# A fused attention and two feed-forward layers on one core: the first batch written out per engine

## What is computed

```
attention, in chunks of 32 queries: context = 8 memory rows + 16 left + 32 own + 8 right
    scores = scale * q_c @ k_full.T ; a = exp(scores - max) / (sum + 1e-9) ; out = a @ v_full
x = out reshaped to 3072 x 512
SOLU layer:  h = x @ w_in (512 x 1024) ; solu = h * softmax(h) ; layer norm * g_ln ; @ w_out (1024 x 512)
second layer: h = x @ w_in2 (512 x 2048) ; g = h * clip(h + 3, 0, 6) / 6 ; @ w_out2 (2048 x 512)
```

## Time and profile before

| | |
|---|---|
| median of 3 runs | 938.34 us (937.13 to 939.4) |
| profiled execution | 938.23 us, span 936.4 us |
| TensorE busy, matmuls | 905.9 us (97%) |
| VectorE, ScalarE, GpSimd busy | 685.4, 473.2, 273.0 us |
| mean granted TensorE clock | 0.985 |
| chain that ended last | TensorE 80%, VectorE 13%, DMA 3%, ScalarE 2% |

### The profile page before, as it was taken

One profiled execution on the slowest core, in us unless ns is written; L12 is line 12 of the kernel. 1 busy time (PEld: TensorE's weight loads), 2 busy tenths in 40 slices (PEclk: granted clock), 3 DMA queues, 4 the chain that ended last, 5 costly groups with the idle time before them and its releaser, 6 DMA issues.

```text
span 936.4 us, 17274 instructions
## 1 busy us (share of the span) xinstructions
PE 905.9 (97%) x6200; PEld 812.0 (87%) x6200; DVE 685.4 (73%) x1094; ACT 473.2 (51%) x1092; POOL 273.0 (29%) x324
## 2 busy tenths in 40 slices
PE   7887999999999999999999999999999999999998
PEld 7666888988888888889988888888799999999997
DVE  3898687878777777866686555555788988878783
ACT  4645465555656564635675555455654333333320
POOL 5452165554432343552002332323550000000000
PEclk8987999999999999999999999999999999999999
DMA  9633326666644476458463333332987434344441
GB/s 191 149 67 63 93 53 178 180 179 171 190 141 137 100 219 165 139 175 334 170 254 128 116 138 123 142 127 111 351 315 270 137 101 149 114 141 135 130 137 45
DMA packets 146907, 146.46 MB, mean 156 GB/s; under 512 B 96936, under 2 KB 107176, under 8 KB 145832
## 3 DMA queue, kind: packets, MB, share of 16 engines
q1 hardware_dynamic: 134328, 100.55, 37.0%
q0 software_dynamic: 7920, 38.94, 11.5%
q10 hardware_dynamic: 4608, 6.29, 1.9%
HBM read 90.05 MB, written 55.71 MB: 156 GB/s over the span
## 4 chain that ended last, share of the span: by engine, by line
PE 80%; DVE 13%; DMA 3%; ACT 2%; issue 2%; SPq 0%; POOL 0%; DVEq 0%; POOLq 0%
PE banks L873 25%; PE banks L916 21%; PE banks L1057 21%; PE banks L827 3%; PE banks L840 2%; PE banks L864 2%; PE banks L796 2%; DVE prob L1317 2%; PE banks L853 2%; DVE gs_raw L1474 2%; DVE gs L1293 2%; DVE small L1313 1%; DMA k_in<-in_k_dram 1%; DMA ws<-w_split_scratch 1%; DVE score L1301 1%
## 5 line engine op out<-in xcount | busy, mean ns | idle before, releaser
L1057 PE MATMUL banks<-vs,gs 128*128 128x256 f32 x2016 | 243.3, 283 | 2.7 <-DVE o_stage L1507 1.5
L1057 PEld LDWEIGHTS banks<-vs,gs 128*128 128x128 f32 x2016 | 242.3, 192 | 3.8 <-DVE o_stage L1507 1.7
L916 PE MATMUL banks<-xs,ws 128*128 128x512 f32 x1008 | 230.5, 390 | 2.4 <-DMA ws<-w_split_scratch 1.8
L916 PEld LDWEIGHTS banks<-xs,ws 128*128 128x128 f32 x1008 | 188.3, 188 | 43.2 <-DMA ws<-w_split_scratch 2.2
L1253 ACT CAST gs<-gs_raw 128x1792 fp32r<-128x1792 f32 x48 | 81.6, 1700 | 132.2 <-DVE gs_raw L1474 132.1
L873 PE MATMUL banks<-y_t,w_out 128*128 128x384 f32 x768 | 140.8, 337 | 0.0
L873 PE MATMUL banks<-w_in,x_t 128*128 128x512 f32 x552 | 133.2, 397 | 1.1 <-DVE solu L1347 1.1
L873 PEld LDWEIGHTS banks<-y_t,w_out 128*128 128x128 f32 x768 | 132.2, 188 | 0.7
L873 PEld LDWEIGHTS banks<-w_in,x_t 128*128 128x128 f32 x552 | 103.1, 190 | 23.1 <-DVE solu L1347 1.4
L1105 ACT ACTIVATE prob<-score,small 96x128 f32<-96x128 f32 x256 | 99.8, 397 | 18.2 <-DVE small L1306 18.2
L1474 DVE TENSOR_TENSOR gs_raw<-gs_raw 128x256 f32<-128x256 f32 x192 | 82.6, 431 | 29.4 <-DMA gs_raw<-g_scratch 24.3
(11 more groups left out here) (88 smaller groups left out, 1077.4 us busy)
## 6 DMA issues: line engine op xcount, KB each, us to landing
g_scratch<-part SPq DMA_DIRECT2D x96, 256.0 KB, 2.0
gs_raw<-g_scratch SPq DMA_DIRECT2D x45, 512.0 KB, 3.9
q_in<-in_q_dram SPq DMA_DIRECT2D x32, 192.0 KB, 3.9
x_scratch<-x_out ACTq DMA_DIRECT2D x32, 192.0 KB, 2.0
out_dram<-o_stage SPq DMA_DIRECT2D x12, 512.0 KB, 5.7
k_in<-in_k_dram SPq DMA_DIRECT2D x24, 240.0 KB
v_in<-in_v_dram SPq DMA_DIRECT2D x24, 240.0 KB
v_split_scratch<-v_split POOLq DMA_DIRECT2D x3, 1792.0 KB, 7.7
```

The source lines that it names most:

```text
L916: mm = pe.matmul(ps, ws[:, W_OF[i], a, kc, :], xs[g][X_OF[i]][:, m, kc, :], start=(fresh and x == 0), stop=(x == len(passes) - 1), skip_gr ...
L1057: mm = pe.matmul(m_ps[i][:, s, :], gs[x][:, a, G_OF[i], s * P:(s + 1) * P], vs[p][:, m, V_OF[i], :], start=(p == 0 and s == 0 and y == 0), ...
```

## The change

Batch 0 no longer goes through `batch(b, first)`. Each engine gets a `first_batch()` with its pieces in an order of its own, by halves of a tile and by quarters of a product (`hidden_part`). Further:

- GpSimd scales the probabilities of attention tiles 0 to 6, one operation per head; later tiles are scaled by VectorE as before.
- All eight weight pieces have a buffer of their own (`w_first`, `w_later`, the latter where `y_t1` lies). GpSimd rounds all eight. VectorE subtracts for w_in 0 to 3. GpSimd subtracts for w_out in four quarters per piece.
- K's window 0 is loaded by ScalarE's queue. The weights and g_ln are asked for once that window is there. ScalarE makes one small copy early.
- `keep_busy` has 8 calls at the start and 8 near the end.
- Q loads wait for the turn of the Q before last, not for K's.

```diff
-        w_raw = at("w_raw", 184, [P, 2, PIECE], F32)
+        w_first = at("w_first", 184, [P, 2, PIECE], F32)
+        w_later = at("w_later", 112, [P, 6, PIECE], F32)
@@ GpSimd
+            def low_weights(p, x):
+                if x == 0:
+                    pool.wait_ge(w_hi_done, p + 1)
+                    pool.wait_ge(w_lo_done, p)
+                cs = slice(x * PIECE // 4, (x + 1) * PIECE // 4)
+                piece = nc.gpsimd.tensor_tensor(w_split_at(p, LO)[:, cs], w_piece(p)[:, cs],
+                                                w_split_at(p, HI)[:, cs].bitcast(F32), ALU.subtract)
+            def scale_half(n, half):
+                pool.wait_ge(srec_done, 2 * n + 1 + half)
+                for h in range(HB * half, HB * (half + 1)):
+                    last = nc.gpsimd.tensor_scalar(prob[:, h, :], prob[:, h, :], srec[:, h:h + 1], 1.0,
+                                                   ALU.mult, ALU.mult)
+                last.then_inc(prob_done, 1)
+            def first_batch():
+                pool.wait_ge(k_in_here[0], kv_here(0, 0))
+                    pool.dma_start(g_ln, moe_g_ln.rearrange("(c p) -> p c", p=P)).then_inc(g_ln_here, 16)
+                load_weights(0)
+                load_weights(1)
+                high_weights(0)
+                high_weights(1)
+                scale_half(0, 0)
+                load_weights(2)
+                scale_half(0, 1)
+                load_weights(3)
+                scale_half(1, 0)
+                scale_half(1, 1)
+                high_weights(2)
+                load_weights(4)
+                high_weights(3)
+                load_weights(5)
+                scale_half(2, 0)
+                scale_weights(4)
+                scale_half(2, 1)
...
+                low_weights(7, 3)
@@ TensorE
+                keep_busy(8)
+                turn_q(0, early_ps[0])
+                turn_k(0, early_ps[1])
+                turn_q(1, early_ps[0])
+                scores(0, True)
...
+                attend(0, 1, False)
+                scores(3, False)
+                hidden_part(0, 0)
+                hidden_part(0, 1)
+                turn_half(2, 0)
+                hidden_part(0, 2)
+                hidden_part(0, 3)
...
+                scores(6, False)
+                turn_half(5, 0)
+                keep_busy(8)
+                turn_half(5, 1)
+                turn_ln_half(1, 0)
+                attend(0, 5, False)
+                turn_ln_half(1, 1)
@@ ScalarE
+                load_window(act, k_in, k, mem_k, k_in_here, 0, 0)
+                act.wait_ge(three_ready, 1)
+                nc.scalar.copy(hsum, three)
+                copy_q(0, early_ps)
@@ VectorE
+            def first_batch():
+                mask_half(0, 0)
+                max_half(0, 0)
+                mask_half(0, 1)
+                low_weights(0)
+                den_half(0, 0)
+                max_half(0, 1)
+                rec_half(0, 0)
+                mask_half(1, 0)
+                max_half(1, 0)
+                den_half(0, 1)
+                rec_half(0, 1)
+                mask_half(1, 1)
+                max_half(1, 1)
+                low_weights(1)
...
+                low_x(0, 0, 0)
+                low_weights(2)
+                max_half(2, 1)
+                low_x(1, 1, 0)
+                low_weights(3)
...
+                low_x(5, 1, 1)
```

More of the change, by code:

```diff
@@ L552, in split_weights, with high_weights @@
+            def high_weights(p):
                 if p < WP1:
-                    hi, lo = (w_in[:, a, p, :] for a in (HI, LO))
+                    pool.wait_ge(w_raw_here[p % 2], 16 * (p // 2 + 1))
                 else:
[L555 to L560, removed]
@@ L726, in batch @@
                         mix_tokens(*{3: (0, 0), 5: (0, 1), 7: (1, 0)}[kk])
[L727 to L737, removed]
+            first_batch()
             batch(1, steps=0)
@@ L875, in split_products, with hidden_part @@
                 return mm
-            def hidden(i, u, par, first):
+            def hidden_part(m, x):
+                half, ks = x // 2, 2 * (x % 2)
+                if x == 0:
+                    if m > 0:
+                        pe.wait_ge(solu_done, m)
+                    pe.wait_ge(x_lo_done, m + 2)
+                if m == 0 and half == 0:
+                    pe.wait_ge(w_lo_done, ks + 2)
+                cols = slice(half * BANK, (half + 1) * BANK)
+                for kc in (ks, ks + 1):
+                    for y, (a, w) in enumerate(((HI, HI), (HI, LO), (LO, HI))):
+                        mm = pe.matmul(h_ps[:, cols], x_t[:, 0, a, kc, m * P:(m + 1) * P], w_in[:, w, kc, cols],
+                                       start=(kc == 0 and y == 0), stop=(kc == KD - 1 and y == 2))
+                if x == 3:
+                    mm.then_inc(h_done, 1)
@@ L1173, in batch @@
+            def batch(b, last=False):
                 for kk in range(TILES):
-                    w = work(kk, first, last)
+                    w = work(kk, last)
                     n = TILES * b + kk - 1
                     i, ii, u = 2 * b + kk // TPG, kk // TPG, kk % TPG
-                    if first and kk < TPG:
-                        copy_qk(kk, early_ps)
-                    if first and kk == 0:
-                        act.wait_ge(w_raw_here[0], 16)
-                        nc.scalar.copy(w_in[:, HI, 0, :], w_raw[:, 0, :]).then_inc(w_hi_done, 1)
@@ L1429, in _ @@
             dve.wait_ge(mask_ready, 1)
-            batch(0, first=True)
+            first_batch()
             with dve.Fori(1, B) as b:
```

635 lines of the change are left out of this document (471 added, 164 removed).

## The result

The changed kernel takes 950.86 us, the median of 4 runs (950.16 to 952.57). The kernel before took 938.85 us beside it (4 runs, 937.13 to 939.4). The ratio is 1.0134, 95% interval 1.0114 to 1.0154: 12 us slower, where 13 us faster was forecast.

A forecast was written before the change was run, and what follows sets the result against it. TensorE bounds after 100 us; before about 92 us VectorE is nearest to the bound. The walk's 19 us less 3 for port waits and 3 for clock give 13 won: 938.2 - 13 = 925 us, range 918 to 934.

The forecast's parts named there:

- after the gauge TensorE is full, so nothing gives the gain back: Rest of the kernel behind the first batch's start-up: all 13 us won earlier would last to the end.
- the gauge: Start of the fourth SOLU tile's product (tile 3) on TensorE, 91.27 us before; its earlier start measures the gain.
- the steady stretch unchanged in length: Sign to check in the dense TensorE part: its duration stays as before.
- The slower one, 944: GpSimd becomes the bound, halves queue behind weight work, all 13 us lost and 6 more; chance 0.09.
- The walk, 19.1 us: Following the five engines' written orders through the first batch up to tile 3's product: 19.1 us won.
- products 0 to 3: TensorE's products of SOLU tiles 0 to 3, walked to start at 28.7, 40.0, 51.1 and 72.2 us.
- Product 3 "near 77": Sign on TensorE: SOLU tile 3's product starts near 77 us with both deductions.
- rival 1: First batch: w_in 0 and 2 land late, or VectorE's subtractions wait for GpSimd; 7 us won, 931; chance 0.18.
- The port waits, 3 us: Deduction before batch 1: small VectorE operations wait for GpSimd at the SBUF port, 3 us, bounds 0 and 8.5.
- the point of failure: Sign on GpSimd: the prediction is wrong if a 96x128 scaling takes 0.5 us or more.
- The clock, 3 us: Deduction for TensorE at half clock over one product, one score set, one turned tile: 3 us, bounds 0 and 14.
- The w_out pieces: GpSimd's last w_out piece ends at 75.7 us, first projection wants it at 79.8: cover of 4 us.

The follow-up runs named there:

- Experiments 1 to 7: Empty instructions or identity passes ahead of the loops of the changed kernel or the one before, or the changed kernel's loop written out: 926.94 to 963.69 us.
- experiment 5: Changed kernel with 16 more keep_busy calls (64 instructions) in TensorE's waits and 24 empty instructions on ScalarE: 926.94 us, ratio 0.9882.
- experiment 7: Changed kernel with batches 1 to 3 written out on SP, TensorE, ScalarE and VectorE instead of looped, no padding: 928.20 us, ratio 0.9896.
- experiment 11: Kernel before with batches 1 to 3 written out on TensorE, VectorE, ScalarE and SP instead of looped: 936.42 us, ratio 0.9984.
- (2): Changed kernel with 32 empty instructions on ScalarE behind its first loads, TensorE unpadded: 943.34 us, ratio 1.0027.
- (1): Changed kernel with 96 empty instructions on TensorE ahead of its first work, ScalarE unpadded: 949.28 us, ratio 1.0100.

## Why the prediction was wrong

**The step that failed** is "after the gauge TensorE is full, so nothing gives the gain back", with its check "the steady stretch unchanged in length". I took the loop's work as unchanged, so its time as constant. The diff changes how many instructions stand ahead of it, 135 fewer for TensorE and 9 more for ScalarE, and that moves the body against the blocks in which it is fetched. Experiments 1 to 7 show it: against 845.1 us behind the gauge the changed kernel takes 23.3 more, but 1.7 more with both bodies moved (5) and 0.8 more without the loop (7). None of my rivals was of this kind. The slower one, 944, had GpSimd as the bound, and that isn't what made this kernel slower. GpSimd is indeed busy 28.1 of the 30 us from 50 to 80, and TensorE waits 8.5 us for its scaled halves before 90 (7.7 us for VectorE's in the kernel before). But the gauge came earlier all the same, and the first projection doesn't wait for it.

**The gain up to the gauge** was sized about right: 11.3 us for 13, from one profile of each kernel. With the code in a good place it also arrives: experiment 7, with the first batch as it is, takes 11.0 us less than the kernel before, and experiment 5, with its added passes, 12.2 us less. That the number came out so near is in part luck, since the terms came out otherwise than I had them:

- *The walk, 19.1 us.* It had products 0 to 3 at 28.7, 40.0, 51.1 and 72.2; measured are 34.60, 45.71, 56.64 and 79.99. The delay is there from the first product on, 5.9, 5.7 and 5.5 us, and 7.8 at the fourth. So the distances from 0 to 2 were right, the way to product 0 and the last stretch weren't. In the last stretch TensorE waits 2.02 us for the turned tile's low part, and its granted clock is 0.66 from 70 to 80 us. (Product 3 "near 77" doesn't fit the sum: 91.3 - 13 is 78.3.)
- *The way to product 0.* w_in 0 is rounded at 14.56, not at 12.9: 1.7 us late. VectorE stands 3.7 us before its subtraction (the column in brackets), which ends at 16.86; the walk had 16.4. Attention tile 1's last maximum ends at 21.76 for 20.6. So the late weights, the front half of rival 1, explain about 1 of the 5.9 us. The rest comes between 22 and 34.6 us: GpSimd's four heads of half 0,1 take 2.92 us beside VectorE's subtraction, 1.41 undisturbed, TensorE waits for them at half clock, and VectorE stands 3.93 us for the scores that come behind. Then comes the subtraction of w_in 2.

```profile
14.56 1.04 POOL L608 CAST w_in<-w_first 128x1024 fp32r<-128x1024 f32 x1 [5.13 <-DMA w_first<-in_moe_w_in_dram]
...
15.63 1.23 DVE L1572 TENSOR_TENSOR w_in<-w_first,w_in 128x1024 fp32r<-128x1024 f32 x1 [3.69 <-POOL w_in L608]
...
20.56 2.92 POOL L623 TENSOR_SCALAR prob<-prob,small 96x128 f32<-96x128 f32 x4
21.68 1.21 DVE L1572 TENSOR_TENSOR w_in<-w_first,w_in 128x1024 fp32r<-128x1024 f32 x1
23.53 0.90 PE L949 MATMUL banks<-ident,prob 96*128 96x96 f32 x4 [2.61 <-POOL prob L623]
...
27.11 0.69 DVE L1581 SCALAR_TENSOR_TENSOR score<-banks,mask 96x512 f32<-96x512 f32 x1 [3.93 <-PE banks L941]
...
30.60 2.85 DVE L1572 TENSOR_TENSOR w_in<-w_later,w_in 128x1024 fp32r<-128x1024 f32 x1 [0.37 <-POOL w_in L608]
31.30 1.05 POOL L608 CAST w_in<-w_later 128x1024 fp32r<-128x1024 f32 x1
```

- *The port waits, 3 us.* The last two lines are the back half of rival 1: the subtraction of w_in 2 takes 2.85 us instead of 1.23 while GpSimd rounds w_in 3, just ahead of product 0. That is 1.6 us; no other of VectorE's four took so long. The small operations, by shape, in 0 to 90 us (busy, mean ns), answer to the earlier trace rows:

```profile
L623 POOL TENSOR_SCALAR prob<-prob,small 96x128 f32<-96x128 f32 x56 | 21.3, 397 | 10.1 <-DVE small L1606 9.8
...
L615 POOL TENSOR_TENSOR w_out<-w_later,w_out 128x256 fp32r<-128x256 f32 x16 | 11.4, 734 | 0.3
...
L1601 DVE TENSOR_SCALAR small<-small 96x4 f32<-96x4 f32 x16 | 6.6, 411 | 1.6 <-ACT prob L1319 1.6
```

  The one that adds 1e-9 fell from 756 to 411 ns, as it should if shorter pieces on GpSimd hold VectorE for less; no run parts the size of the pieces from the new order. A head's scaling takes 397 ns, where I had taken 300, and a half 1.5 us on the mean (21.3 us over 14) instead of 1.2. The head stays below the 0.5 us that I had named as the point of failure. A quarter of w_out takes 734 ns, for 0.6.
- *The clock, 3 us.* Its mean of 10 to 90 us stayed at 0.84, but the mean hides where it is low. From 10 to 30 us it was 0.53, where the kernel before had 0.83, and TensorE was busy 11.9 us instead of 15.8; scores took 2.02 us there, and from 30 to 70 us, through products 0 to 2, it was 1.00. So the low clock lay on the way to product 0, not at the products. Sixteen more calls in the gaps (experiment 5) raised it to 0.79 in 10 to 30 us and to 0.93 in 10 to 90, and product 0 came 2.1 and the gauge 3.0 us earlier. That this is the clock's doing is likely, but the gauge is one profile's. Kernel before, changed kernel and experiment 5, then experiment 5's longer window:

```profile
10.00:30.00 20.00, 15.83 (x147) 13.95 (x149) 15.24 (x24) 12.15 (x44) 14.00 (x11) 0.83 0.98 202
10.00:30.00 20.00, 11.88 (x83) 9.49 (x83) 11.41 (x22) 9.86 (x40) 11.07 (x21) 0.53 0.75 167
10.00:30.00 20.00, 15.03 (x132) 12.94 (x134) 12.41 (x23) 11.62 (x44) 12.83 (x23) 0.79 0.80 181
10.00:90.00 80.00, 68.99 (x554) 57.62 (x556) 58.98 (x119) 51.04 (x182) 55.05 (x101) 0.93 0.59 130
```

- *The w_out pieces* were in time: the last ended at 81.8 us, and the first projection came at 87.20, cover of 5.4 us (4 forecast).

**What stays open.** That 1044, 1005 and 973 are good positions for TensorE and 909, 941 and 1140 bad ones is measured, as 165, 198 and 206 good and 174 bad for ScalarE. Why these is argued. TensorE's body touches 7 or 8 blocks of 256 instructions by where it begins, ScalarE's 3 or 4 of 128. That the smaller number stays and the larger doesn't agrees with all ten positions if the loaded program of each engine begins with 59 to 67 instructions that the compiled one doesn't show; I worked that number out from these positions, and no run tests it. Nor did I test how long the wait is without transfers beside it: in 180 to 190 us the DMA engines are busy 0.99 of the time, and a block fetched there may take longer than it must. And why K 1 came 1.3 us earlier and the clock was higher in experiment 11's profile, with the first batch unchanged, isn't known.

## What to carry to other kernels

When the time of a stretch that a change doesn't touch changes, look at the waits with the releaser "issue" and at the packets of the instruction queues before anything else: here 18 and 10 blocks more came with 23 us lost. In these runs a loop body as long as this one ran again without a fetch only from some positions, so an edit ahead of it, one that does nothing included, could move the time by 2% in either direction. So compare the time ahead of the loop and the time behind it separately, the first over more than one profile, and judge an edit with its bodies well placed or with the loop written out, which cost nothing here in either kernel.

## What the runs showed of the hardware

- A jump back to a body that is refetched cost 10 to 12 us in the changed kernel: TensorE stood two or three times, mostly 3.3 to 3.8 us each, ScalarE beside it once, 5.1 and 7.1 us, and the granted clock was 0.57 to 0.70 in the windows around it. With TensorE's body alone refetched (2) the part behind the gauge was 19 us longer than in the kernel before, with ScalarE's alone (1) 16.
- Straight code with 44 and 24 blocks fetched has no such wait (experiment 7).
- An empty TensorE instruction that counts a semaphore took about 0.15 us (14.27 idle us for a row of 96). The 16 calls of `keep_busy` that did the same for the placement lay in idle time and cost nothing at the gauge.
